# Output matmuls of a mixture-of-experts kernel: rows of four of a kind in place of two kinds in turns

## The reference

```python
# layer 1 (layer 2 is the same with a sigmoid gate beside the softmax, and without the skip and the residual)
do_compute = x @ w_skip > 0
e_idx = argmax(xc @ w_gate)              # one expert for each row
h = np.maximum(xc[mask] @ w1[e], 0.0)    # 192 -> 1024
y[mask] = gate_w[mask, None] * (h @ w2[e])   # 1024 -> 192
out[do_compute] = xc + y
```

## Time and profile before

| what | value |
|---|---|
| median of 3 runs | 1185.56 us |
| the profiled execution's own time | 1185.56 us |
| its span (first to last instruction) | 1183.8 us |
| PE busy, PEld busy | 1133.7 us (96%), 1035.2 us (87%) |
| DVE, ACT, POOL busy | 659.2, 512.6, 403.1 us |
| L1104 PE, 1488 matmuls | mean 364 ns |
| L1111 PE, 1488 matmuls | mean 255 ns |
| mean granted TensorE clock | 0.980 of full |

### The profile page before, as it was taken

The page is one execution under the profiler, slowest core; times in us unless marked ns, Lnnn a source line. Parts: engine busy times, 40 slices in busy tenths (PEclk is TensorE's granted clock), DMA queues, the critical chain, the costliest instruction groups (busy, mean ns, idle before and its releaser), DMA issues.

```text
span 1183.8 us, 30936 instructions
## 1 busy us (share of the span) xinstructions
PE 1133.7 (96%) x8638; PEld 1035.2 (87%) x8639; DVE 659.2 (56%) x2070; ACT 512.6 (43%) x1190; POOL 403.1 (34%) x435
## 2 busy tenths in 40 slices
PE   7999984999999999999889999999999999999997
PEld 5656553999999999999779999999999999999997
DVE  2445554577777777777635454454545445454443
ACT  2545551343434444444334454443444444354443
POOL 3477776132323333333313223231323223223212
PEclk9999997899999999999989999999999999999999
DMA  6854424332423233342343242332424233222221
GB/s 184 235 151 150 121 76 127 108 101 76 106 71 110 80 94 94 91 109 82 83 142 89 84 110 77 109 86 81 113 81 119 68 99 93 67 63 71 68 67 51
DMA packets 137313, 118.11 MB, mean 100 GB/s; under 512 B 40963, under 2 KB 131977, under 8 KB 137296
## 3 DMA queue, kind: packets, MB, share of 16 engines
q1 hardware_dynamic: 107424, 69.69, 22.5%
q0 software_dynamic: 15328, 27.96, 7.0%
q10 hardware_dynamic: 14544, 20.28, 6.1%
HBM read 86.72 MB, written 33.08 MB: 101 GB/s over the span
## 4 chain that ended last, share of the span: by engine, by line
PE 85%; issue 6%; POOL 5%; DMA 2%; DVE 1%; ACT 1%; SPq 0%; POOLq 0%; DVEq 0%; ACTq 0%
PE bank L1088 30%; PE bank L1104 25%; PE bank L1111 12%; PE bank L1079 5%; POOL buckets L429 5%; PE bank L1028 2%; PE bank L1049 2%; PE bank L1029 2%; PE bank L936 1%; PE bank L1048 1%; PE bank L1011 1%; PE bank L1012 1%; PE bank L1037 1%; DMA buckets<-rows,slot_i 1%; PE bank L1038 1%
## 5 line engine op out<-in xcount | busy, mean ns | idle before, releaser
L1104 PE MATMUL bank<-w,hh 128*128 128x384 f32 x1488 | 449.6, 364 | 0.0
L1111 PE MATMUL bank<-w,hl 128*128 128x192 f32 x1488 | 363.9, 255 | 0.0
L800 DVE SCALAR_TENSOR_TENSOR hl<-bank,hh 128x512 fp32r<-128x512 f32 x372 | 252.6, 689 | 131.8 <-ACT hh L596 125.3
L596 ACT ACTIVATE hh<-bank 128x512 fp32r<-128x512 f32 x372 | 221.4, 598 | 175.5 <-PE bank L1088 168.2
L1111 PEld LDWEIGHTS bank<-w,hl 128*128 128x128 f32 x1488 | 284.0, 192 | 0.0
L1104 PEld LDWEIGHTS bank<-w,hh 128*128 128x128 f32 x1488 | 280.8, 189 | 0.0
L455 POOL DMA_INDIRECT out<-y_rows,out_i x120 | 117.3, 977 | 439.9 <-DVE out_i L878 407.6
L1088 PE MATMUL bank<-xAh,w1h 128*128 128x256 f32 x744 | 221.4, 298 | 0.0
L1088 PE MATMUL bank<-xB,w1h 128*128 128x256 f32 x744 | 209.9, 282 | 0.0
L1088 PE MATMUL bank<-xAl,w1h 128*128 128x256 f32 x744 | 209.1, 281 | 0.0
L1088 PE MATMUL bank<-xAh,w1l 128*128 128x256 f32 x744 | 208.0, 280 | 0.0
(11 more groups left out here) (157 smaller groups left out, 1383.6 us busy)
## 6 DMA issues: line engine op xcount, KB each, us to landing
xprep<-buckets SPq DMA_DIRECT2D x95, 192.0 KB, 2.9
xkeep<-buckets ACTq DMA_DIRECT2D x93, 196.0 KB, 2.5
raw<-w_all SPq DMA_DIRECT2D x56, 192.0 KB
xwin<-x SPq DMA_DIRECT2D x12, 768.0 KB
raw<-w_all SPq DMA_DIRECT2D x56, 128.0 KB
raw<-w_all SPq DMA_DIRECT2D x112, 64.0 KB
xprep<-buckets SPq DMA_DIRECT2D x95, 64.0 KB, 2.5
xwin<-x SPq DMA_DIRECT2D x5, 672.0 KB
```

The costliest lines, as they stand in the source:

```text
L596: nc.scalar.activation(hh[:, 2 * c:2 * c + 2, :].rearrange("p c t -> p (c t)"), bank[c][:], ACT.Relu).then_inc(s["h_high"], 1)
L800: nc.vector.scalar_tensor_tensor(hl[:, 2 * c:2 * c + 2, :].rearrange("p c t -> p (c t)"), bank[c][:], 0.0, h, ALU.max, ALU.subtract).then_ ...
L1104: return nc.tensor.matmul(bank[Y[h]][:, 0:2 * D], hh[:, j, t], w2[:, par, j, :, :].rearrange("p a d -> p (a d)"), start=(j == 0), stop=(j ...
L1111: last = nc.tensor.matmul(bank[Y[h]][:, 0:D], hl[:, j, t], w2[:, par, j, 0, :], start=False, stop=False)
```

## The change

The loop over the eight chunks j becomes a loop over the four pairs c, with the same wait at its head. In each pair the four high matmuls are split in two rows of two (both halves of j = 2c at the start, both halves of j = 2c + 1 at the end), and the four low matmuls stand between them. Over the border from pair to pair, two highs at the end and two at the start make a row of four.

```diff
-                            for j in range(FC):
-                                if j % 2 == 0:
-                                    pe.wait_ge(s["h_low"], g * PAIRS + (j // 2 + 1))
-                                for h in range(SUB):
-                                    t = slice(h * 128, (h + 1) * 128)
-
-                                    def high_terms():
-                                        return nc.tensor.matmul(
-                                            bank[Y[h]][:, 0:2 * D], hh[:, j, t],
+                            for c in range(PAIRS):
+                                pe.wait_ge(s["h_low"], g * PAIRS + (c + 1))
+
+                                def high_terms(j):
+                                    for h in range(SUB):
+                                        done = nc.tensor.matmul(
+                                            bank[Y[h]][:, 0:2 * D], hh[:, j, h * 128:(h + 1) * 128],
                                             w2[:, par, j, :, :].rearrange("p a d -> p (a d)"),
                                             start=(j == 0), stop=(j == FC - 1))
-
-                                    if j == 0:
-                                        high_terms()
-                                    last = nc.tensor.matmul(bank[Y[h]][:, 0:D], hl[:, j, t], w2[:, par, j, 0, :],
-                                                            start=False, stop=False)
-                                    if j > 0:
-                                        last = high_terms()
-                                if m == 0 and j == 5:
+                                    return done
+
+                                high_terms(2 * c)
+                                for j in (2 * c, 2 * c + 1):
+                                    for h in range(SUB):
+                                        nc.tensor.matmul(bank[Y[h]][:, 0:D], hl[:, j, h * 128:(h + 1) * 128],
+                                                         w2[:, par, j, 0, :], start=False, stop=False)
+                                last = high_terms(2 * c + 1)
+                                if m == 0 and c == 2:
                                     ranks(g)
                             last.then_inc(s["y_ready"], 1)
```

## The result

The changed kernel takes 1189.47 us (median of 8 runs, 1188.0 to 1190.38) against 1186.0 us for the kernel before (8 runs, 1185.22 to 1189.61). The ratio is 1.0024, with a 95% interval of 1.0012 to 1.0035: slower by 2.8 us, between 1.4 and 4.2 (the two medians are 3.5 us apart). The forecast was 1184.6 us, in a range that ended at 1189.0.

What follows compares the result with a forecast made beforehand. TensorE itself was taken to bound both passes. The order inside tiles gave -1.0 us, banks, waits and the tile's end 0; with the 1183.8 us span and 1.76 us outside it, 1184.6 us, range 1177 to 1189.

Steps and rivals of the forecast that it cites:

- What bounds the kernel: Both passes: TensorE itself, busy 96% of the span; changes between a tile's matmuls reach the end almost one to one.
- Step (1): Order of the 32 output-layer matmuls in a tile: 990 changed places over all tiles at -1 ns, so -1.0 us.
- x + y - p: Slot of high behind high (0.173 us) plus low behind low (0.113) minus one high and one low in turns (0.287): -1 ns.
- kind-only reading: Output-layer slots depend only on whether a matmul is high or low, so any order costs the same: difference zero.
- The sign: Whole kernel: slightly faster, by 1.0 us; chance 0.30 of faster by over 0.2%, 0.14 of slower by over 0.2%.
- Step (2): Output layer, neighbouring matmuls now all in different banks: cost 0.
- Step (3): Waits for `h_low` before each pair: more than 2 us to spare, cost 0.
- Step (4): From a tile's last high to the next tile's load: nothing changes; bounds +2.2 us and -5.6 us.
- rival B: Tile's end timed from the last high's start: each of 93 tiles 0.024 us longer, 1187.8 us; chance 0.14.
- Rival A: Output layer: turning between kinds costs time, high behind high takes 0.1625 us; -11.4 us, 1174.2 us; chance 0.28 with halves.
- the rule of the Trainium skill: Full matmul streams: columns over 2.4 GHz and 2.5 ns each, 162.5 ns for a high's 384 columns.
- Rival C: Output layer: next load not hidden, high behind high keeps 0.20 us; +25.7 us, 1211 us; chance 0.05 with anything like it.

Runs made afterwards that it cites:

- the crossed order: Kernel before, low and high still in turns, but each high adds to the other bank than the low in front of it: 9.633 us a tile of pass 1.
- the exchanged lows: Changed kernel with two of the lows trading places, so that lows add two by two to the same bank: 9.680 us a tile of pass 1.

## Why the prediction was wrong

- **What bounds the kernel**: right. TensorE alone, no new wait, and a nanosecond in a tile's slots goes through to the end: 0.047 us x 59 and 0.007 x 31 are 3.0 us, timed 2.8 (1.4 to 4.2).
- **Step (1), the difference of a tile is 11 x (x + y - p)**: this is the step that failed. It counts the places where like stands behind like and puts all else in the tile at nothing, without a reason. The places themselves went as the kind-only reading says: from the second of a row on, a high to the next took 171 to 182 ns (176 in the mean) and a low to the next 107 to 115 (111), and whole rounds in pass 1 took exactly as long as with turns, x + y - p = 0. The 47 ns lie elsewhere: 21 in L1088, whose slot went from 116.7 to 117.8 ns, 3 in L1079, and 23 in the output layer, about 20 of them within its first ten matmuls (an estimate, 1598 ns against 1515 with turns, which have one high less and one low more, 61 to 65 ns by x - y). No term of the sum could hold that, and its range of "some 3 ns together" was a statement on the rows' resolution, not on whether the slots of other instructions stay. In pass 0 the sum came nearly true: 0.007 us, all of it in the output layer.
- **The sign**: the 1 ns that I took off came from one distance read to 10 ns. It had no weight, and "faster" got 0.30 by it. The fiftieth part of a distance over fifty tiles was to be had in the same view.
- **Step (2), banks**: right (the crossed order, 9.633 us, and the exchanged lows, 9.680).
- **Step (3), the waits for `h_low`**: right, PE never waits for it in the changed kernel.
- **Step (4), the tile's end, and rival B**: the end went as the forecast had it, L1079 0.267 us behind the last high's listed start (0.26 forecast, 0.28 with B). The distance from the first high's load to the load of L1079 went from 4.784 to 4.808 us, inside the 0.03 that the forecast allowed itself, so this sign couldn't tell. One reason given for the end doesn't hold: in the earlier trace rows the next pair with 128 rows, 440.41 to 440.74, takes 0.33 us as well, so the 0.22 and 0.32 us are no price of a change of rows. The mechanism of B isn't there. Two highs at the end add 0.007 us to turns, where B wanted 0.024. The output layer of a tile did get longer by 0.023 us, near B's number, and B's time (1187.8) is near the measured one, but both by luck: 0.02 us more lie in L1088, which B doesn't touch, and pass 0, with the same two highs at its end, lost 0.007 us.
- **Rival A and the rule of the Trainium skill ("TensorE: Matmul & The Clock Gate", section "Back-to-back issue gap")**: a full stream of highs at 162.5 ns would have made the tile shorter by 0.13 us. The trace disagrees: a high behind a high took 176 ns in the mean, and no order of likes gained more than 0.007 us in pass 1. The section itself calls the columns over 2.4 GHz and 2.5 ns the gap of an isolated matmul, and says that at large sizes it comes out too long for a stream of weight loads and matmuls; here it came out too short. Rival C is refuted by the same numbers.
- **What stays open**: why this sequence of kinds (two highs, then rows of four, two highs at the end) slows L1088 by 1% and the start of the output layer, 0.5% of a tile of pass 1 together, while the same with its last four matmuls in turns, with lows first, or with rows of eight leaves L1088 alone, and why pass 0 is spared. Excluded by runs: the banks, the level of an execution, the tile's end by itself, the rows by themselves, and a position that a 0.1 us shift would end. The granted clock shows nothing (1.00 before and after). A cause inside TensorE was not reached.

## What to carry to other kernels

Where an engine is busy all the time, measure a loop by one instruction in two iterations that lie fifty apart: this gave 1 ns where the timeline has 10, repeated over several groups of runs and told orders apart that the total time couldn't. Don't take the slots of unchanged instructions in such a loop for fixed when the order beside them changes; an order of equal work moved the tile from 9.627 to 9.680 us, with costs that didn't add. Where the total surprises, cut the tile into pieces: 0.007 us in sum can be 0.018 more in one and 0.011 less in the others. So an order of matmuls is chosen by trying several, and a forecast for one should leave 0.5% either way.

## What the runs showed of the hardware that I had not expected

- Slots of matmuls can slow down together: L1088 at 116.7 to 116.8 ns in twelve profiles and at 117.8 in the eight with the changed order in pass 1, without a wait and at the same granted clock.
- Tile times came in steps: 9.627, 9.633, 9.640, 9.653, 9.680 and 9.773 us, 11.473, 11.500 and 11.507, all whole multiples of 6.67 ns within the reading. The doubled transpose with turns (9.737) is no exception: its tiles are 9.730 and 9.743 us in turn, 19.473 for two, which is a multiple again. Why there is such a step isn't shown.
- A semaphore instruction in the middle of TensorE's stream cost nothing (9.633 with and without).
